# Eight slots of a fused attention and feed-forward kernel: second product in three rounded passes instead of plain float32

## The reference, cut to what matters

```python
q_p, k_p = phi(q), phi(k)                        # products of two sketches, 64 features per head
x = (q_p @ (k_p.T @ v)) / (q_p @ z + 1e-6)
u = x + real(fft(fft(x, axis=1), axis=2))
un = (u - mean(u)) / sqrt(var(u) + 1e-6)
x = u + relu(un @ w_ch1) @ w_ch2                 # layer 1: 128 -> 512 -> 128
h = relu(x @ w_in)                               # 128 -> 1024
gate = sigmoid(conv over 3 tokens (h))
out = (h * gate) @ w_out                         # 1024 -> 128
```

## Time and profile before

| | |
|---|---|
| median of 3 runs | 265.8 us (265.61 to 266.71) |
| profiled execution | 265.86 us, its span in the trace 264.1 us |
| granted TensorE clock | 1.00 |
| PE busy | 250.1 us (95%), 1524 matmuls |
| DVE busy | 219.2 us (83%), 388 instructions |
| ACT busy | 185.9 us (70%), 357 instructions |
| POOL busy | 27.0 us (10%) |

### The profile page before, as it was taken

One profiled execution on the slowest core, in us unless ns is written; L12 is line 12 of the kernel. 1 busy time (PEld: TensorE's weight loads), 2 busy tenths in 40 slices (PEclk: granted clock), 3 DMA queues, 4 the chain that ended last, 5 costly groups with the idle time before them and its releaser, 6 DMA issues.

```text
span 264.1 us, 4307 instructions
## 1 busy us (share of the span) xinstructions
PE 250.1 (95%) x1524; PEld 210.8 (80%) x1524; DVE 219.2 (83%) x388; ACT 185.9 (70%) x357; POOL 27.0 (10%) x90
## 2 busy tenths in 40 slices
PE   8999999999999999998679999998999999999985
PEld 6989999989989989977567777776778677777753
DVE  0747978997998779795779989988799999998992
ACT  2351436333487454667989998999899989978872
POOL 0000000001513333238200000000000000000000
PEclk9999999999999999999999999999999999999999
DMA  6959730300000000000000000002000002002002
GB/s 191 388 206 350 282 95 0 93 4 0 2 0 2 1 1 2 0 2 2 0 0 0 2 0 0 1 2 84 0 0 2 0 0 84 5 0 84 0 0 84
DMA packets 4341, 13.04 MB, mean 49 GB/s; under 512 B 736, under 2 KB 1504, under 8 KB 4320
## 3 DMA queue, kind: packets, MB, share of 16 engines
q1 hardware_dynamic: 4320, 12.77, 13.2%
HBM read 10.54 MB, written 2.23 MB: 48 GB/s over the span
## 4 chain that ended last, share of the span: by engine, by line
PE 75%; ACT 13%; DVE 6%; issue 4%; ACTq 0%; DVEq 0%
PE ps L584 19%; PE ps L505 8%; PE ps L507 8%; PE ps L506 8%; PE ps L498 6%; PE ps L422 6%; PE ps L434 5%; ACT arena L773 4%; PE ps L463 4%; PE ps L545 3%; PE ps L447 3%; ACT arena L781 3%; ACT arena L786 2%; PE ps L590 2%; PE ps L484 2%
## 5 line engine op out<-in xcount | busy, mean ns | idle before, releaser
L584 PE MATMUL ps<-arena,wout 128*128 128x364 f32 (+1 forms) x192 | 62.8, 468 | 0.7 <-DVE arena L1005 0.7
L584 PEld LDWEIGHTS ps<-arena,wout 128*128 128x128 f32 x192 | 35.9, 189 | 20.8 <-issue 2.8
L993 DVE SCALAR_TENSOR_TENSOR arena<-arena,taps 128x1088 f32<-128x1088 f32 x32 | 43.2, 1349 | 4.5 <-ACT arena L781 4.5
L998 DVE SCALAR_TENSOR_TENSOR arena<-arena,taps 128x1088 f32<-128x1088 f32 x32 | 43.2, 1350 | 0.1
L773 ACT ACTIVATE arena<-ps 128x364 f32<-128x364 f32 x96 | 40.0, 479 | 3.8 <-PE ps L507 3.4
L1005 DVE TENSOR_TENSOR arena<-arena 128x1088 f32<-128x1088 f32 (+2 forms) x36 | 41.4, 1161 | 1.4 <-ACT arena L786 1.2
L505 PE MATMUL ps<-x2hi,wlo 128*128 128x364 f32 x96 | 38.8, 404 | 3.6 <-ACT arena L773 3.2
L781 ACT ACTIVATE arena<-arena,taps 128x1088 f32<-128x1088 f32 x32 | 38.7, 1209 | 0.6
L786 ACT ACTIVATE arena<-arena 128x1088 f32<-128x1088 f32 x32 | 35.5, 1111 | 1.9 <-DVE arena L998 1.9
L506 PE MATMUL ps<-x2lo,whi 128*128 128x364 f32 x96 | 31.5, 329 | 0.0
L507 PE MATMUL ps<-x2hi,whi 128*128 128x364 f32 x96 | 31.5, 328 | 0.0
(11 more groups left out here) (81 smaller groups left out, 420.0 us busy)
## 6 DMA issues: line engine op xcount, KB each, us to landing
arena<-v_d SPq DMA_DIRECT2D x4, 594.0 KB, 3.7
arena<-qT_d SPq DMA_DIRECT2D x3, 545.0 KB, 7.2
arena<-kT_d SPq DMA_DIRECT2D x3, 544.5 KB, 6.3
out_d<-arena SPq DMA_DIRECT2D x3, 544.0 KB, 2.7
cos_t<-cos_d SPq DMA_DIRECT2D x1, 926.5 KB, 5.6
sin_t<-sin_d SPq DMA_DIRECT2D x1, 926.5 KB, 7.4
arena<-qT_d SPq DMA_DIRECT2D x2, 272.5 KB, 4.6
wraw<-w_d SPq DMA_DIRECT2D x2, 256.0 KB, 5.4
```

Of the source, the lines that this page charges most:

```text
L584: pe.matmul(ps[:, OUT_BANK + t, 0:z - a], wout[:, c, :], gate[:, i % GATES, a:z], start=(c == 0), stop=(c == C2 - 1)).then_inc(wout_done, 1)
L993: dve.scalar_tensor_tensor(out=gate[:, i % GATES, 1:S + 1], in0=h2[:, i % HIDDENS, 0:S], scalar=taps[:, i % C2, 0:1], in1=gate[:, i % GATE ...
L998: dve.scalar_tensor_tensor(out=gate[:, i % GATES, 1:S + 1], in0=h2[:, i % HIDDENS, 2:S + 2], scalar=taps[:, i % C2, 2:3], in1=gate[:, i % ...
```

## The change

The ten slots 22 to 31 stay plain; the eight slots 32 to 39 get a low half again, and their second products are done in three passes. `lows(n)` is the number of low halves that have been made once slot n has its own, since the semaphore `h1lo_ready` no longer counts one per slot.

```diff
-LOW_UNTIL = NC1 // 2 + 2
+LOW_UNTIL, LOW_FROM = NC1 // 2 + 2, 32
...
         def has_low(n):
-            return n < LOW_UNTIL
+            return n < LOW_UNTIL or n >= LOW_FROM
+
+        def lows(n):
+            return n + 1 if n < LOW_UNTIL else LOW_UNTIL + max(0, n + 1 - LOW_FROM)
...
                 if has_low(n):
-                    claim(bank_h1(n), (h1hi_ready, n + 1), (h1lo_ready, n + 1))
+                    claim(bank_h1(n), (h1hi_ready, n + 1), (h1lo_ready, lows(n)))
                 else:
                     claim(bank_h1(n), (h1hi_ready, n + 1))
...
                 if has_low(n):
-                    pe.wait_ge(h1lo_ready, n + 1)
+                    pe.wait_ge(h1lo_ready, lows(n))
                     three_pass(ps[:, bank, 0:G1], whi[:, w:w + 128], wlo[:, w:w + 128], h1hi[:, n % 3, :], h1lo[:, n % 3, :],
                                False, c == C1 - 1).then_inc(w2_done, 1)
                 else:
```

## The result

| | kernel before | changed kernel |
|---|---|---|
| median of 20 runs each | 266.44 us (265.56 to 267.06) | 267.01 us (266.24 to 268.19) |
| ratio | | 1.0031, 95% interval 1.0017 to 1.0045 |
| forecast | | 266.4 us (265.0 to 268.0), +0.6 |
| profiled execution: time, span | 265.86, 264.1 us | 268.11, 266.3 us |
| mean granted TensorE clock in it | 1.000 | 0.987 |

The account below looks back on a forecast made before the run. TensorE and VectorE were both taken as full where the change acts, and both set the end. TensorE's +0.51 sets the last left tap; with 0.1 for hand-overs, +0.6 gives 266.4 us, range 265.0 to 268.0.

Parts of the forecast that it names:

- Savings on TensorE, 0.13 us a slot: Second products of the eight slots: three rounded passes take 0.60 us instead of 0.73, together 1.04 us saved.
- Cost on VectorE, 0.52 and not 0.61: Each added low half delays VectorE's successors by 0.52 us, not its whole 0.61; eight cost 4.2 us, counting 0.52.
- Rival D: VectorE's low halves count whole durations instead of start distances: about +0.9 or +1.0 at the end, 266.8; chance 0.12.
- Slots 32 and 33 at nothing: Their low halves fall into VectorE's gaps and add nothing; with no gap, 1.04 us on VectorE only.
- The wait in slot 34, +0.60: Slot 34's transposes wait for VectorE's low half to free PSUM bank 2; all three engines 0.60 us later.
- The stall at `up(39)`, 0.82: TensorE waits 0.82 us before up(39) for slot 38's low half, which reads the bank it needs.
- The gaps that give back: VectorE's gaps at mixed rows absorb 0.69 and 0.44 us; the product at 242.70 cuts its shift from 2.07 to 0.74.
- The base: Starting time of the kernel before: a median of 265.8 us, with the profiled execution 0.06 above it.
- A: Low halves stay hidden: slot 34's half ends in time, up(39) doesn't stall; 265.7 us, chance 0.12.
- B: The change pays in full: TensorE's 1.04 us arrive at the end, 264.8 us; chance 0.06 together with E.
- E: Three passes following a slot's other work don't run at 0.20 us each; chance 0.06 together with B.
- C: VectorE's lateness isn't handed back at 242.70 but turns round through ScalarE's sigmoids: +1.8, 267.6, or +2.9, 268.7; chance 0.20.

Follow-up runs that it names:

- no32: The changed kernel with slot 32 plain again, slots 33 to 39 keeping low halves and rounded passes; ratio 1.0045 to the kernel before.
- no34: The changed kernel with slot 34 plain, so its transposes wait for ScalarE's copy alone; ratio 0.9992 to the kernel before.
- dve_only: The changed kernel's eight low halves and bank waits, but second products of slots 32 to 39 left plain float32; ratio 1.0046 to the kernel before.

## Why the prediction was right, and where it was not

- **Savings on TensorE, 0.13 us a slot.** Held: in the trace after the three passes of a second product start at 195.33 and give way at 195.93, and the passes alone bring 0.90 us, where 7 x 0.13 = 0.91 had been expected to arrive.
- **Cost on VectorE, 0.52 and not 0.61.** Held. The low half at 171.76 is followed at 172.29, again before its recorded end. Timeline of VectorE after:

```profile
171.76 0.61 DVE L942 SCALAR_TENSOR_TENSOR h1lo<-ps,h1hi 128x436 fp32r<-128x436 f32 x1
172.29 1.28 DVE L1008 TENSOR_TENSOR arena<-arena 128x1088 f32<-128x1088 f32 x1
```

  Rival D is out. The section "The DRAIN you can't avoid" of the Trainium skill's page "VectorE: DVE Perf Modes", by which whole durations count, doesn't describe this pair; the exception that it names does.
- **Slots 32 and 33 at nothing.** Right for VectorE. But slot 32's saving of 0.13 us, rightly called swallowed by the wait of slot 34, was not harmless: it lengthened TensorE's idle time from 1.75 to 1.88 us, and two dips in one run appeared only with 1.87 or more.
- **The wait in slot 34, +0.60.** +0.65 measured, and shown to be the main cause by taking slot 34 out (+0.02) and by doing it alone (+0.49).
- **The stall at `up(39)`, 0.82.** In the profile of the changed kernel it isn't there: `up(39)` starts at 206.88, straight behind the hidden chunk's last pass (timeline of TensorE):

```profile
206.71 0.33 PE L510 MATMUL ps<-x2hi,whi 128*128 128x364 f32 x1
206.88 0.36 PE L508 MATMUL ps<-unhi,wlo 128*128 128x436 f32 x1
```

  The prediction lists just that as a sign of being wrong, and taken alone it would have made the step look wrong. It is there, with brackets of 0.74, 0.58 and 0.20 us, in the three kernels that have slot 38's half and no dip behind slot 34 (`no32`, `no34`, `dve_only`). With the dip, TensorE is so late that the half is ready: from the transposes (186.74) to the next projection (L587, 191.36) it takes 4.62 us, against 3.33 before (185.04 to 188.37); 0.13 was saved in between, so the low clock costs 1.42. TensorE's shift is then 0.65 - 0.13 + 1.42 = 1.94, less three savings 1.55 at `up(39)` (measured 1.58 from the anchor), less three more 1.16 at the end (measured 1.18). The dip takes 1.4 us of TensorE, but only about 0.5 of the time (+1.18 against +0.70), for it takes the place of the stall.
- **The gaps that give back.** Held: the gap before the product closed, and TensorE, not VectorE, arrives last at the end. In the profile of `no32` VectorE's lateness from the anchor goes the way of the sum: 2.55 behind slot 39's half (forecast 2.51), 2.10 behind the mixed rows (2.07), 0.77 behind the product (0.74), 0.70 at the last left tap (0.51, or 0.6 with the 0.1 for hand-overs).
- **The step that was missing.** No term for the clock. The sum without it, +0.6, meets the runs at full clock (+0.78, three runs) and the clean trace (+0.70) within 0.2. Over all runs the changed kernel had ratios of 1.0031, 1.0041 and 1.0058, 0.8 to 1.5 us, and what lies over 0.7 goes with the dip: its runs with two dips take 267.6 to 267.7 on average, 1.3 over those at full clock. A first dip cancels in the ratio if it comes as often in both kernels: 51 of 92 runs of the kernel before have one (mean 266.4 against 265.54). Where it lies in them only profiles could tell; in the six profiles of this study that have an early one it is near 133 us, at an idle time of 2.52 us that all kernels have. That the first ratio came out as low as 0.8 us was luck in part: of the 20 runs of before in it 14 took longer than 265.94, the slowest run of before at full clock, so that the early dip was in more of them than usual; against the 92 later ones the same 20 runs of the changed kernel are 1.1 us slower on average.
- **The base.** The median of before over 20 runs is 266.44, not the 265.8 of the three runs shown. 265.8 lay near the runs at full clock; the 0.6 by which the changed kernel's median exceeds the forecast is the size of this shift.

Rivals: A (265.7) fell, the wait in slot 34 is in every profile of the changed kernel and that at `up(39)` in the clean one. B fell with A, and E by the passes 0.20 us apart. C fell: in the profile of the changed kernel only ScalarE's last sigmoid, at 258.99, waits for a right tap, as before. Its place was well chosen, though: in the kernel with six slots, where TensorE and ScalarE are early, the sigmoid at 209.97 waits 0.39 us for VectorE, and nothing comes of it.

How often the dip behind slot 34 comes can only be estimated. With an idle time of 1.87 us or more there, 32 of 56 runs had two dips, 19 one and 5 none. The early dip lies ahead of the change; if it comes in 51 of 92 runs here too, about 31 of the 56 have it, so nearly all of these have the late one as well, and most of the 19 single dips are late ones (both profiles with a single one say so): an estimate of some 50 in 56, not 32. The times fit: the changed kernel's 16 runs with one dip average 266.84, 0.5 over its three at full clock, what the traces give for a late dip, and not 0.8, what the early one costs the kernel before.

What stays open is why the dip needs the last 0.13 us of idle time: none of 172 runs with 1.75 us or less had two dips, and between `no32` and the changed kernel nothing else differs behind the wait. (A late dip alone can't be told from an early one there by the count; none of the eight profiles with 1.75 us or less has one.) That the two are tied is shown; how the chip decides isn't, and the slots, products and halves of the other kernels were changed along with the idle time.

## What to carry to other kernels

A second reader of a buffer is a new wait for whoever writes the buffer next, even if the diff adds no wait to that writer: list the next claimants, and skip those that come at once (here two slots of eight carried the whole loss, and the rest was a gain of 0.25% to 0.31%). A saving ahead of a wait only lengthens the wait, and a longer idle TensorE can come back at half the clock. Compare profiles from an anchor just ahead of the change, and look at the clock of each run before blaming the code behind it.

## What the runs showed of the hardware

TensorE fell to half its clock (granted 0.50) at idle times of 1.87 to 2.52 us: behind slot 34 in the five profiles that have so long a one there, near 133 us in six of thirteen. The fall came between 0.6 us before the end of the idle time and 1.4 us after it, and each of the eleven dips lasted 3.4 us. Whether the early one comes doesn't seem to be decided near 133 us: by the clock records of the traces the clock first rises to full between 5.5 and 7.2 us from the span's start in the six profiles that have it, and between 4.0 and 5.4 in the seven that don't. The passes show the dip in the timeline of TensorE after, those of 364 columns every 0.30 us and those of 436 every 0.36, and a few us later the 436 ones every 0.20:

```profile
188.27 0.51 PE L508 MATMUL ps<-x2hi,wlo 128*128 128x364 f32 x1
188.57 0.51 PE L509 MATMUL ps<-x2lo,whi 128*128 128x364 f32 x1
188.88 0.51 PE L510 MATMUL ps<-x2hi,whi 128*128 128x364 f32 x1
189.18 0.57 PE L508 MATMUL ps<-unhi,wlo 128*128 128x436 f32 x1
189.54 0.57 PE L509 MATMUL ps<-unlo,whi 128*128 128x436 f32 x1
...
195.33 0.36 PE L508 MATMUL ps<-h1hi,wlo 128*128 128x436 f32 x1
195.53 0.36 PE L509 MATMUL ps<-h1lo,whi 128*128 128x436 f32 x1
```

The Trainium skill describes such a gate in "TensorE: Matmul & The Clock Gate", section "What's actually happening": the low level is the default and activity lifts it; the trace agrees in the levels, 0.50 and 1.00. I had not expected it from so short an idle time in an engine that is 95% busy.
